# Scores of the first two tiles in free PSUM banks, tile 0 loaded in halves, and a new order of the first tiles

## The chip, the cores and the metric

The kernel runs on one core of one Trainium2 chip. The metric is the device time of one execution in microseconds. Engines are named as in the profile: PE (TensorE), DVE (VectorE), ACT (ScalarE), POOL (GpSimd), SP (the queue that issues most loads).

## The reference

Attention over 12 tiles of 128 queries (2 batches, 8 heads of 64, 6 tiles of a sequence of 768), where each query sees 8 global keys and the 96 positions up to its own, with a bias by distance; then a block with a softmax-like gate and a norm; then a block with SiLU:

```python
scores = scale * q @ k.T + bias            # masked by global and local windows
a = exp(scores - max); a = a / (sum(a) + 1e-9)
x = a @ v                                  # 1536 tokens x 512
h = x @ w_in                               # 512 -> 1024
e = exp(h - max(h)); solu = h * e / (sum(e) + 1e-9)
x = ((solu - mean) / sqrt(var + 1e-6) * g_ln) @ w_out     # 1024 -> 512
h = x @ w2_in                              # 512 -> 2048
out = (h * sigmoid(h)) @ w2_out            # 2048 -> 512
```

## The kernel before

Each engine has its own program, written out by hand, and the engines are tied by semaphores. A tile of 128 queries sees 232 keys (8 global, 96 before, its own 128). The eight heads form four pairs, so each step of attention exists four times per tile: `step(t, p)` for tile t and pair p. Where fp32 operands go through fast matmuls, they are split into a high and a low part (`_hi`, `_lo`), and three matmuls make one product.

For a tile of the attention the chain is: loads of keys and queries; on PE `early_scores(t, half)`, which makes two of the four pairs, four matmuls into the banks `score_ps[0]` and `score_ps[1]`; on DVE `mask(t, p)`, which adds the bias tables and finds the maximum; on ACT `exps(t, p)`; on DVE the reciprocals of the sums; on ACT or POOL `normalise`; on PE `turn_probs(t, p)` (four transposes); on ACT or DVE `copy_probs_t(t, p)`, out of the single bank `probs_t_ps`; on PE `values(t, p)` into `x_t_ps`. Then ACT's `x_high` and DVE's `x_low` split the result, and PE makes the hidden product: `hidden_by_rows(t, k)` for the first two tiles (six matmuls of 512 columns for each of four k, so that each needs one piece of `w_in` only), `hidden(t, n)` afterwards. On that follow `hidden_max` (DVE), `hidden_exp` (ACT), `hidden_solu` (DVE), `square` (ACT), `rstd` (POOL), `norm_u` (POOL or DVE), then on PE `turn_u(t, r)`, `project(t, r)`, and `turn_x1(t)`; `copy_x1` and `x1_high` are ACT's copies around it.

The bias tables of batch tile 0 come from ACT (`first_table(p)`), those of the other tiles from POOL (`late_table(p)`, four bias operations for two calls). Weights `w_in` and `w_out` are split in eight pieces: `split_w(n)` on ACT and DVE, `split_in_high(n)` and `low_w(n)` on POOL.

Before the regular loop `step(i)`, i from 4 on, each engine runs `first_steps()`, a list of such calls for tiles 0 to 3 and parts of tile 4 in a fixed order. An engine takes its list strictly in order, so a call that waits holds everything behind it. Each engine also has one branch, on a flag that is read from memory (`wide_flag`): a general path for other window sizes, not taken here. PE starts with `keep_warm`, matmuls on zeros whose result nobody reads.

SP issues the loads in order: tile 0's, tile 1's, values, `w_in` pieces, then, behind the branch, tile 2 (waits for the scores of tile 0), two pieces of `w_out`, tile 3 (waits for the scores of tile 1), two more, tile 4, values of tile 2, and the first loads of tile 5. ACT's queue issues half of tile 0's.

## Time and profile before

| | us |
|---|---|
| median of three runs | 494.79 (494.17 to 496.78) |
| the profiled execution | 493.58 |
| its span, first to last instruction | 491.5 |
| PE busy | 483.5 (98%) |
| DVE, ACT, POOL busy | 302.4, 269.7, 224.4 |

The timed runs and the profiled one are different executions of the same program. The span leaves out what lies before the first and after the last instruction of the program, 2.1 us here. Busy time of PE includes matmuls that overlap with the next one, so that the time from one start to the next tells more than the duration of one.

### The profile page before, as it was taken

The numbers are of one execution on the slowest core, as the hardware profiler recorded it, in microseconds if no ns is written. First come the engines' busy times: TensorE is split into PE (matmuls) and PEld (weight loads), VectorE is DVE, ScalarE is ACT, GpSimd is POOL, SyncE is SP. The second block draws the span as 40 slices with busy tenths as digits, with TensorE's granted clock in tenths as the row PEclk, the third lists the DMA queues.
The fourth block names the chain that finished last, engine by engine and source line by source line (L and its number), as shares of the span: only waits on it lengthen the run. The fifth ranks groups of instructions, "written<-read, shape, count | busy, mean of one in ns | idle before, by whom it ended". The sixth has DMA issues, their size and how long they took to land.

```text
span 491.5 us, 8017 instructions
## 1 busy us (share of the span) xinstructions
PE 483.5 (98%) x2761; PEld 414.2 (84%) x2761; DVE 302.4 (62%) x731; ACT 269.7 (55%) x598; POOL 224.4 (46%) x293
## 2 busy tenths in 40 slices
PE   8999999999999999999999999999999999999997
PEld 5667888888888878888898999988899998988995
DVE  5788665575675786666565667564565546545542
ACT  4988656576476465645845444455454454344422
POOL 6624207788778788530624422444135431444100
PEclk9999999999999999999999999999999999999999
DMA  8991021633532532302222202220116202220003
GB/s 239 299 260 49 18 66 37 159 82 79 159 101 61 159 105 57 125 0 87 86 87 87 82 6 85 85 87 31 55 65 237 86 4 83 87 85 1 1 1 128
DMA packets 20202, 44.38 MB, mean 90 GB/s; under 512 B 2560, under 2 KB 8128, under 8 KB 20160
## 3 DMA queue, kind: packets, MB, share of 16 engines
q1 hardware_dynamic: 20000, 43.47, 29.4%
q8 instruction: 23, 0.38, 0.3%
q10 hardware_dynamic: 160, 0.37, 0.3%
q14 instruction: 19, 0.16, 0.1%
HBM read 40.69 MB, written 3.15 MB: 89 GB/s over the span
## 4 chain that ended last, share of the span: by engine, by line
PE 68%; POOL 18%; issue 4%; DVE 4%; DMA 3%; ACT 1%; SPq 1%; POOLq 0%; DVEq 0%; ACTq 0%
PE hidden_ps L1162 24%; PE score_ps L1185 9%; POOL k_split L687 6%; PE x_ps L995 6%; POOL probs L714 5%; PE x_t_ps L1185 5%; PE x_ps L1185 5%; PE probs_t_ps L1185 5%; PE turn_ps L1185 4%; PE hidden_ps L950 3%; POOL k_split L685 3%; DVE solu L1738 2%; POOL q_lo L701 2%; DMA w_out_raw<-w_out 2%; PE score_ps L892 2%
## 5 line engine op out<-in xcount | busy, mean ns | idle before, releaser
L853 POOL TENSOR_TENSOR wo_lo<-w_raw,wo_hi 128x512 fp32r<-128x512 f32 x32 | 41.4, 1313 | 145.6 <-ACT wo_hi L1434 145.6
L1446 ACT ACTIVATE act_hi<-mix_c 128x384 fp32r<-128x384 f32 x64 | 33.7, 526 | 96.5 <-DVE mix_c L1827 96.2
L714 POOL TENSOR_SCALAR probs<-probs,exp_inv 128x232 f32<-128x232 f32 x80 | 35.4, 460 | 51.7 <-DVE exp_inv L1597 48.6
L1265 ACT ACTIVATE probs<-logits,low_logit 128x232 f32<-128x232 f32 x96 | 45.5, 478 | 3.4 <-DVE low_logit L1584 2.7
L1827 DVE TENSOR_TENSOR mix_u<-hidden_ps,mix_p 128x384 f32<-128x384 f32 x16 | 8.9, 558 | 57.0 <-PE hidden_ps L1162 57.0
L995 PE MATMUL x_ps<-w_out_hi,u_hi 128*128 128x512 f32 x96 | 40.6, 423 | 0.0
L1832 DVE TENSOR_TENSOR act_lo<-mix_c,act_hi 128x384 fp32r<-128x384 f32 x64 | 36.1, 566 | 6.3 <-ACT mix_c L1447 5.5
L995 PE MATMUL x_ps<-w_out_hi,u_lo 128*128 128x512 f32 x96 | 38.0, 395 | 0.0
L995 PE MATMUL x_ps<-w_out_lo,u_hi 128*128 128x512 f32 x96 | 37.5, 390 | 0.0
L1584 DVE CUSTOM_DVE_ANT_0 logits<-score_ps,bias 128x232 f32<-128x232 f32 x96 | 33.5, 395 | 2.3 <-issue 2.3
L950 PE MATMUL hidden_ps<-w_in_hi,x_hi 128*128 128x512 f32 x80 | 33.1, 414 | 0.0
L1447 ACT ACTIVATE mix_c<-mix_c 128x384 f32<-128x384 f32 x64 | 32.6, 509 | 0.0
L950 PE MATMUL hidden_ps<-w_in_hi,x_lo 128*128 128x512 f32 x80 | 31.5, 394 | 0.0
L950 PE MATMUL hidden_ps<-w_in_lo,x_hi 128*128 128x512 f32 x80 | 31.2, 390 | 0.0
L903 PE MATMUL probs_t_ps<-identity,probs 128*116 128x128 f32 x192 | 29.2, 274 | 0.2 <-ACT probs_t L1272 0.2
L1798 DVE TENSOR_TENSOR wa_lo<-w_sums,wa_hi 128x1024 fp32r<-128x1024 f32 x16 | 19.6, 1224 | 13.7 <-ACT wa_hi L1426 13.7
L903 PEld LDWEIGHTS probs_t_ps<-identity,probs 128*116 128x116 f32 x192 | 22.1, 134 | 6.6 <-issue 2.3
L1613 DVE TENSOR_TENSOR u_lo<-turn_ps,u_hi 128x512 fp32r<-128x512 f32 x24 | 16.5, 688 | 18.1 <-ACT u_hi L1279 18.1
L1162 PE MATMUL hidden_ps<-late_x_hi,wa_lo 128*128 128x384 f32 x80 | 27.1, 339 | 0.0
L1162 PE MATMUL hidden_ps<-late_x_hi,wa_hi 128*128 128x384 f32 x80 | 27.0, 337 | 0.0
L1162 PE MATMUL hidden_ps<-late_x_lo,wa_hi 128*128 128x384 f32 x80 | 27.0, 337 | 0.0
L1311 ACT ACTIVATE expd<-hidden_ps,stat 128x1024 f32<-128x1024 f32 x12 | 13.4, 1115 | 24.5 <-DVE stat L1651 24.5
(205 smaller groups left out, 1456.4 us busy)
## 6 DMA issues: line engine op xcount, KB each, us to landing
w_raw<-w SPq DMA_DIRECT2D x16, 1024.0 KB, 4.9
v_sb<-v_win SPq DMA_DIRECT2D x22, 224.0 KB
late_k_raw<-k_t SPq DMA_DIRECT2D x16, 232.0 KB, 4.0
k_raw<-k_t SPq DMA_DIRECT2D x14, 232.0 KB, 3.6
out<-out_sb SPq DMA_DIRECT2D x12, 256.0 KB, 2.1
w_in_raw<-w_in SPq DMA_DIRECT2D x4, 512.0 KB, 6.8
w_out_raw<-w_out SPq DMA_DIRECT2D x4, 512.0 KB, 10.5
late_q_raw<-q_t SPq DMA_DIRECT2D x16, 128.0 KB, 3.9
```

What stands on the lines that cost most here:

```text
L714: last = nc.gpsimd.tensor_scalar(probs[p][:, e, :], probs[p][:, e, :], exp_inv[:, p, e:e + 1], 0.0, ALU.mult, ALU.add)
L853: nc.gpsimd.tensor_tensor(wo_lo[j % 2][:, c, :], w2_raw[j % 2][:, c, BANK:2 * BANK], wo_hi[j % 2][:, c, :].bitcast(F32), ALU.subtract).the ...
L903: last = nc.tensor.transpose(probs_t_ps[0:HALF_KEYS, n * P:(n + 1) * P], probs[p][:, e, c * HALF_KEYS:(c + 1) * HALF_KEYS], identity[:, :])
L950: last = nc.tensor.matmul(hidden_ps[:, n * BANK:(n + 1) * BANK], x[:, k * P:(k + 1) * P], w[:, k, n * BANK:(n + 1) * BANK], start=(k == 0 ...
L995: last = nc.tensor.matmul(x1_ps[:, :], u[:, c * P:(c + 1) * P], w[:, c, :], start=(c == 0 and m == 0), stop=(c == KF - 1 and m == 2))
L1162: last = nc.tensor.matmul(dst, w[b][:, w_slot, cols], x[:, k, :], start=(k == 0 and m == 0), stop=(k == 1 and m == 2))
L1185: last = nc.tensor.matmul(out_ps[n][:, :], a[c][:, i * P:(i + 1) * P], w[b][:, chunk, :], start=(opens and m == 0), stop=(closes and m == 2))
L1265: last = nc.scalar.activation(probs[p][:, e, :], logits[b][:, e, :], ACT.Exp, scale=-1.0, bias=low_logit[:, b, e:e + 1], accum_out=exp_sum ...
L1446: nc.scalar.activation(act_hi[c][:, :], mix_c[c][:, :], ACT.Silu)
L1447: nc.scalar.activation(mix_c[c][:, :], mix_c[c][:, :], ACT.Silu).then_inc(act_hi_done, 1)
L1584: last = nc.vector.tensor_tensor_reduce(logits[b][:, e, :], score_ps[b][:, e * KEYS:(e + 1) * KEYS], bias[0 if t % TILES_PER_BATCH == 0 el ...
L1832: nc.vector.tensor_tensor(act_lo[c][:, :], mix_c[c][:, :], act_hi[c][:, :].bitcast(F32), ALU.subtract).then_inc(act_lo_done, 1)
```

## The change

1. `early_scores` writes to `score_bank(t, p)`. For tiles 0 and 1 the eight pairs go to eight places: the two score banks, `x_t_ps`, `x1_ps`, the two halves of `hidden_ps`, and the score banks again. The scores of tile 1, half 0, wait for no mask; those of half 1 wait for the first two masks. Waits for masks now stand before the first real use of the borrowed banks (`values(0, 0)`, `hidden_by_rows(0, 0)`, `project(0, 0)`). The warm-ups write to `turn_ps`.
2. `load_first` loads tile 0 in two halves of columns, from SP and from ACT, eight transfers in place of four, with a semaphore for each half.
3. `mask(0, 1)` stands in front of DVE's branch, `early_scores(0, 1)` in front of PE's. POOL's fill of the far part of the bias is divided: two heads early, six behind the flag.
4. The warm-ups start on a quarter of the zeros, made by POOL: five matmuls of 128 columns, then seven of 512 instead of nine; later 8 in place of 14, two of which had been full fp32.
5. All engines get a new order for the first tiles. Some steps change their engine: `norm_u(2)` goes from DVE to POOL; high parts of `w_in` 0 and 2 go from ACT to POOL; low parts of 0 and 1 from POOL to DVE, of 3 from DVE to POOL; copies and normalisations of some pairs swap.

Of DVE's new list the diff below shows only the ends.

```diff
+    early_score_ps = [*score_ps, x_t_ps, x1_ps, hidden_ps[:, 0:BANK], hidden_ps[:, BANK:2 * BANK], *score_ps]
...
+    def score_bank(t, p):
+
+        return early_score_ps[PAIRS * t + p] if t < 2 else score_ps[p % 2]
...
-    ACT_NORMALISES = ((0, 0), (0, 1), (1, 2), (1, 3), (2, 3), (3, 0), (3, 2), (3, 3))
-    POOL_NORMALISES = ((0, 2), (0, 3), (1, 1), (1, 0), (2, 0), (2, 1), (2, 2), (3, 1))
-    ACT_WEIGHTS = (2, 0, 3, 4, 5, 6, 7)
-    POOL_WEIGHTS = (1,)
-    POOL_LOWS = (0, 1)
+    ACT_NORMALISES = ((0, 0), (1, 1), (1, 2), (2, 2), (3, 1), (3, 3))
+    POOL_NORMALISES = ((0, 1), (0, 2), (0, 3), (1, 0), (1, 3), (2, 0), (2, 1), (2, 3), (3, 0), (3, 2))
+    ACT_WEIGHTS = (3, 4, 5, 6, 7)
+    POOL_WEIGHTS = (0, 2, 1)
+    POOL_LOWS = (3,)
...
+    def load_first(eng, unit):
+
+
+        rows = slice(unit * DH, unit * DH + DH)
+        for half, loaded in enumerate((first_half_loaded, early_loaded[0])):
+            keys = slice(half * 2 * KEYS, (half + 1) * 2 * KEYS)
+            queries = slice(half * 2 * P, (half + 1) * 2 * P)
+            eng.dma_start(staged_k_raw[rows, keys], k_v[0, unit][:, keys]).then_inc(loaded, 16)
+            eng.dma_start(staged_q_raw[rows, queries], q_v[0, unit][:, queries]).then_inc(loaded, 16)
...
-            load_early(0)
+            load_first(sp, 1)
             load_early(1)
...
+            nc.gpsimd.memset(x_hi[:, 0:P].bitcast(F32), 0.0).then_inc(first_zeros_made, 1)
...
-            nc.gpsimd.memset(bias[0][:, :, 0:BEFORE], -BIG / SCALE).then_inc(far_made, 1)
+            nc.gpsimd.memset(bias[0][:, 0:2, 0:BEFORE], -BIG / SCALE).then_inc(far_made, 1)
...
             flag()
+            nc.gpsimd.memset(bias[0][:, 2:HEADS, 0:BEFORE], -BIG / SCALE).then_inc(far_made, 1)
             with pool.If(wide_flag(pool) > 0):
...
             late_distances()
+            normalise(0, 1)
             late_table(0)
             late_table(1)
+            normalise(0, 2)
+            split_in_high(0)
+            normalise(0, 3)
             late_table(2)
             late_table(3)
-            normalise(0, 2)
+            normalise(1, 0)
+            split_in_high(2)
             split_in_high(1)
-            normalise(0, 3)
-            normalise(1, 1)
-            normalise(1, 0)
-            low_w(0)
-            low_w(1)
+            low_w(3)
+            normalise(1, 3)
             normalise(2, 0)
             normalise(2, 1)
-            normalise(2, 2)
+            normalise(2, 3)
+            normalise(3, 0)
             rstd(0)
             norm_u(0)
-            normalise(3, 1)
+            normalise(3, 2)
+            rstd(1)
+            normalise(4, 0)
             normalise(4, 1)
-            normalise(4, 0)
-            rstd(1)
             rstd(2)
+            norm_u(2)
...
-                if half == 0:
+                if t == 0 and half == 0:
+                    pe.wait_ge(first_half_loaded, 64)
+                elif t == 0 or half == 0:
                     pe.wait_ge(early_loaded[t], 64)
-                after(pe, masked_done, PAIRS * t + 2 * half)
+                if t > 1:
+                    pe.wait_ge(masked_done, PAIRS * t + 2 * half)
+                elif (t, half) == (1, 1):
+                    pe.wait_ge(masked_done, 2)
...
-                        last = nc.tensor.matmul(score_ps[unit][:, e * KEYS:(e + 1) * KEYS], queries[rows, h * P:(h + 1) * P],
+                        dst = score_bank(t, 2 * half + unit)[:, e * KEYS:(e + 1) * KEYS]
+                        last = nc.tensor.matmul(dst, queries[rows, h * P:(h + 1) * P],
...
+                if (t, p) == (0, 0):
+                    pe.wait_ge(masked_done, 3)
...
+                if t == 0 and k == 0:
+                    pe.wait_ge(masked_done, PAIRS + 2)
...
+                    if t == 0 and r == 0:
+                        pe.wait_ge(masked_done, PAIRS)
...
+                    nc.tensor.matmul(turn_ps[:, :], x_hi[:, 0:P], x_hi[:, :], start=True, stop=True)
...
-                keep_warm(2)
-                keep_warm_whole(2)
-                early_scores(0, 1)
-                keep_warm(8)
+                keep_warm(4)
+                early_scores(1, 0)
+                early_scores(1, 1)
                 turn_probs(0, 0)
-                keep_warm(2)
-                early_scores(1, 0)
+                keep_warm(4)
                 turn_probs(0, 1)
                 values(0, 0)
                 turn_probs(0, 2)
-                early_scores(1, 1)
                 values(0, 1)
                 turn_probs(0, 3)
                 values(0, 2)
                 values(0, 3)
                 turn_probs(1, 0)
+                turn_probs(1, 1)
+                hidden_by_rows(0, 0)
                 early_scores(2, 0)
-                turn_probs(1, 1)
                 values(1, 0)
-                hidden_by_rows(0, 0)
+                values(1, 1)
                 hidden_by_rows(0, 1)
+                early_scores(2, 1)
+                turn_probs(1, 2)
                 hidden_by_rows(0, 2)
                 hidden_by_rows(0, 3)
-                turn_probs(1, 2)
-                early_scores(2, 1)
-                values(1, 1)
                 turn_probs(1, 3)
+                early_scores(3, 0)
+                turn_probs(2, 0)
                 values(1, 2)
                 values(1, 3)
-                turn_probs(2, 0)
-                early_scores(3, 0)
+                early_scores(3, 1)
                 turn_probs(2, 1)
+                values(2, 0)
+                turn_probs(2, 2)
+                values(2, 1)
                 hidden_by_rows(1, 0)
-                values(2, 0)
-                early_scores(3, 1)
+                values(2, 2)
+                turn_probs(2, 3)
                 hidden_by_rows(1, 1)
-                values(2, 1)
-                turn_probs(2, 2)
+                turn_probs(3, 0)
+                values(2, 3)
+                turn_u(0, 0)
+                turn_probs(3, 1)
                 hidden_by_rows(1, 2)
-                turn_probs(2, 3)
-                values(2, 2)
                 hidden_by_rows(1, 3)
-                turn_u(0, 0)
-                values(2, 3)
-                turn_probs(3, 0)
+                turn_u(0, 1)
+                turn_probs(3, 2)
                 early_scores(4, 0)
-                turn_u(0, 1)
+                turn_probs(3, 3)
                 project(0, 0)
-                turn_probs(3, 1)
+                all_values(3)
                 project(0, 1)
-                turn_probs(3, 2)
                 hidden(2, 0)
-                turn_probs(3, 3)
+                turn_u(1, 0)
                 hidden(2, 1)
-                turn_u(1, 0)
-                all_values(3)
                 turn_u(1, 1)
                 project(1, 0)
-                early_scores(4, 1)
                 turn_x1(0)
                 project(1, 1)
+                early_scores(4, 1)
...
+            pe.wait_ge(first_zeros_made, 1)
+            for _ in range(5):
+                nc.tensor.matmul(turn_ps[:, 0:P], x_hi[:, 0:P], x_hi[:, 0:P], start=True, stop=True)
             pe.wait_ge(zeros_made, 1)
-            keep_warm(9)
+            keep_warm(7)
             early_scores(0, 0)
+            early_scores(0, 1)
...
 
                 first_table(2)
+                first_table(3)
                 exps(0, 1)
-                first_table(3)
                 early_normalise(0, 0)
                 exps(0, 2)
-                early_normalise(0, 1)
                 exps(0, 3)
                 copy_probs_t(0, 1)
                 exps(1, 0)
+                copy_probs_t(0, 2)
                 exps(1, 1)
-                split_w(2)
-                split_w(0)
-                split_w(3)
+                copy_probs_t(0, 3)
+                early_normalise(1, 1)
                 exps(1, 2)
                 x_high(0)
+                split_w(3)
+                copy_probs_t(1, 1)
                 exps(1, 3)
                 split_w(4)
                 exps(2, 0)
+                early_normalise(1, 2)
                 exps(2, 1)
                 split_w(5)
-                early_normalise(1, 2)
-                early_normalise(1, 3)
+                exps(2, 2)
+                copy_probs_t(1, 2)
+                copy_probs_t(1, 3)
+                exps(2, 3)
+                hidden_exp(0)
+                x_high(1)
+                early_normalise(2, 2)
+                copy_probs_t(2, 1)
+                exps(3, 0)
+                exps(3, 1)
+                square(0)
+                early_normalise(3, 1)
+                exps(3, 2)
+                exps(3, 3)
+                copy_probs_t(3, 0)
+                early_normalise(3, 3)
+                u_high(0, 0)
                 split_w(6)
-                hidden_exp(0)
-                copy_probs_t(1, 3)
-                exps(2, 2)
-                x_high(1)
-                copy_probs_t(2, 0)
-                exps(2, 3)
-                exps(3, 0)
-                early_normalise(2, 3)
-                copy_probs_t(2, 1)
                 split_w(7)
-                square(0)
-                copy_probs_t(2, 2)
-                exps(3, 1)
-                exps(3, 2)
-                early_normalise(3, 0)
-                u_high(0, 0)
                 x_high(2)
+                copy_probs_t(3, 2)
+                u_high(0, 1)
                 hidden_exp(1)
-                u_high(0, 1)
-                exps(3, 3)
+                copy_probs_t(3, 3)
                 exps(4, 0)
+                square(1)
                 exps(4, 1)
-                early_normalise(3, 2)
-                early_normalise(3, 3)
-                square(1)
                 copy_x1(0)
-                copy_probs_t(3, 2)
                 u_high(1, 0)
-                hidden_exp(2)
                 x_high(3)
                 u_high(1, 1)
+                hidden_exp(2)
+                x1_high(0)
                 square(2)
-                x1_high(0)
                 copy_x1(1)
...
-            act.dma_start(staged_k_raw[0:DH, :], k_v[0, 0]).then_inc(early_loaded[0], 16)
-            act.dma_start(staged_q_raw[0:DH, :], q_v[0, 0]).then_inc(early_loaded[0], 16)
+            load_first(act, 0)
...
-            nc.vector.memset(x_hi[:, :].bitcast(F32), 0.0).then_inc(zeros_made, 1)
+            nc.vector.memset(x_hi[:, P:BANK].bitcast(F32), 0.0).then_inc(zeros_made, 1)
...
-                norm_u(2)
                 x1_low(0)
...
             mask(0, 0)
+            mask(0, 1)
             with dve.If(wide_flag(dve) > 0):
```

PE behind its branch, up to the first product with values. The banks and `probs_63` to `probs_66` (pairs 0 to 3) are named with their buffer numbers. Before:

```order
L1034 MATMUL x_ps<-x_hi 128x512 x2
L1039 MATMUL x_ps<-x_hi 128x512 x2
L892 MATMUL score_ps<-staged_k_raw,staged_q_raw 128x232 x4
L1034 MATMUL x_ps<-x_hi 128x512 x8
L903 MATMUL probs_t_ps<-identity,probs_63 116x128 x4
L1034 MATMUL x_ps<-x_hi 128x512 x2
L892 MATMUL score_ps<-next_k_raw,next_q_raw 128x232 x4
L903 MATMUL probs_t_ps<-identity,probs_64 116x128 x4
L937 MATMUL x_t_ps<-probs_t_67,v_sb_59 64x128 x4
```

and now:

```order
L1067 MATMUL turn_ps<-x_hi 128x512 x4
L919 MATMUL hidden_ps<-next_k_raw,next_q_raw 128x232 x4
L919 MATMUL score_ps<-next_k_raw,next_q_raw 128x232 x4
L930 MATMUL probs_t_ps<-identity,probs_63 116x128 x4
L1067 MATMUL turn_ps<-x_hi 128x512 x4
L930 MATMUL probs_t_ps<-identity,probs_64 116x128 x4
L966 MATMUL x_t_ps<-probs_t_67,v_sb_59 64x128 x4
L930 MATMUL probs_t_ps<-identity,probs_65 116x128 x4
L966 MATMUL x_t_ps<-probs_t_68,v_sb_60 64x128 x4
```

The scores of tile 0's second half are gone from here (they stand ahead of the branch), all scores of tile 1 stand ahead of the first turn, and eight warm-ups are left of fourteen.

ACT at the end of its list, from the exponential of tile 2's hidden row (`expd,stat<-hidden_ps`) on; `expd,stat<-solu` is `square(2)`, `x_f` and `own_x_hi` are the two operations of `x1_high(0)`, `x_sb` is `copy_x1`. Before:

```order
L1311 ACTIVATE expd,stat<-hidden_ps,stat 128x1024
L1307 ACTIVATE x_hi<-x_t_ps 128x512
L1279 ACTIVATE u_hi<-turn_ps 128x512
L1316 ACTIVATE expd,stat<-solu,stat 128x1024
L1391 ACTIVATE x_f_118<-turn_ps 128x4x128
L1393 ACTIVATE own_x_hi<-turn_ps 128x4x128
L1382 ACTIVATE x_sb<-x_ps 128x512
```

and now (the list shown begins with `u_high(1, 0)`):

```order
L1308 ACTIVATE u_hi<-turn_ps 128x512
L1336 ACTIVATE x_hi<-x_t_ps 128x512
L1308 ACTIVATE u_hi<-turn_ps 128x512
L1340 ACTIVATE expd,stat<-hidden_ps,stat 128x1024
L1420 ACTIVATE x_f_118<-turn_ps 128x4x128
L1422 ACTIVATE own_x_hi<-turn_ps 128x4x128
L1345 ACTIVATE expd,stat<-solu,stat 128x1024
L1411 ACTIVATE x_sb<-x_ps 128x512
```

`square(2)` stood ahead of `x1_high(0)` and now stands behind it; both `u_high` of tile 1 now stand ahead of the exponential.

POOL at the same place, around the entry of the regular loop; `stat<-stat` pairs are `rstd`, the rows into `solu` are `norm_u`. Before:

```order
L714 TENSOR_SCALAR probs_64<-probs_64,exp_inv 128x232 x4
L714 TENSOR_SCALAR probs_63<-probs_63,exp_inv 128x232 x2
L722 TENSOR_SCALAR stat<-stat 128x1
L724 TENSOR_TENSOR stat<-stat 128x1
L722 TENSOR_SCALAR stat<-stat 128x1
L724 TENSOR_TENSOR stat<-stat 128x1
L714 TENSOR_SCALAR probs_65<-probs_65,exp_inv 128x232 x2
L714 TENSOR_SCALAR probs_66<-probs_66,exp_inv 128x232 x2
```

and now:

```order
L730 TENSOR_SCALAR probs_63<-probs_63,exp_inv 128x232 x2
L730 TENSOR_SCALAR probs_64<-probs_64,exp_inv 128x232 x2
L738 TENSOR_SCALAR stat<-stat 128x1
L740 TENSOR_TENSOR stat<-stat 128x1
L804 TENSOR_TENSOR stat<-stat 128x1
L805 TENSOR_TENSOR stat<-stat 128x1
L807 TENSOR_SCALAR solu<-solu,stat 128x1024
L730 TENSOR_SCALAR probs_65<-probs_65,exp_inv 128x232 x2
L730 TENSOR_SCALAR probs_66<-probs_66,exp_inv 128x232 x2
```

`norm_u(2)`, with its two small operations, has come in front of tile 4's pairs 2 and 3.

## Rows read from the trace of the kernel before

**Rows 1.** The page: PE's share, then two groups (count, busy us, mean ns).

```profile
PE 483.5 (98%) x2761; PEld 414.2 (84%) x2761; DVE 302.4 (62%) x731; ACT 269.7 (55%) x598; POOL 224.4 (46%) x293
...
L1265 ACT ACTIVATE probs<-logits,low_logit 128x232 f32<-128x232 f32 x96 | 45.5, 478 | 3.4 <-DVE low_logit L1584 2.7
...
L1584 DVE CUSTOM_DVE_ANT_0 logits<-score_ps,bias 128x232 f32<-128x232 f32 x96 | 33.5, 395 | 2.3 <-issue 2.3
```

**Rows 2.** Busy us of each engine by stretch, then clock, DMA share and GB/s.

```profile
0.00:24.44 24.44, 21.32 (x130) 14.15 (x130) 15.93 (x76) 16.72 (x52) 16.72 (x42) 1.00 0.97 269
24.44:72.44 48.00, 46.98 (x310) 36.53 (x309) 36.08 (x112) 34.21 (x87) 11.17 (x22) 1.00 0.38 94
72.44:200.00 127.56, 126.89 (x863) 106.67 (x862) 84.14 (x259) 76.64 (x202) 100.77 (x122) 1.00 0.38 102
```

**Rows 3.** Waits of PE: who waited for whom, us in total, times, longest.

```profile
PE x_t_ps L937 <- ACT probs_t L1272: 1.0, 1, 1.0
...
PE score_ps L877 <- POOL q_lo L701: 0.4, 2, 0.2
```

**Rows 4.** Timeline to 24.5 us: start, us, engine, line, operation, count, idle before it.

```profile
1.46 4.21 PE L1034 MATMUL x_ps<-x_hi 128*128 128x512 f32 x9 [1.46 <-DVE x_hi L1526]
...
5.96 1.78 PE L892 MATMUL score_ps<-staged_k_raw,staged_q_raw 64*128 64x232 f32 x8 [0.30 <-DMA staged_q_raw<-q_t]
...
7.91 0.06 DVE L1582 MEMSET wait_mark<- 128x1 f32 x1 [2.00 <-PE score_ps L892]
...
9.79 0.06 DVE L1582 MEMSET wait_mark<- 128x1 f32 x1 [1.11 <-issue]
...
11.60 2.12 PE L1034 MATMUL x_ps<-x_hi 128*128 128x512 f32 x8
...
20.80 0.66 PE L937 MATMUL x_t_ps<-probs_t,v_sb 116*64 116x128 f32 x8 [0.45 <-DVE probs_t L1609]
...
24.44 0.50 PE L965 MATMUL hidden_ps<-w_in_hi,x_hi 128*128 128x512 f32 x1
```

**Rows 5.** DMA view of the first 50 us: issues, KB, us from issue to landing.

```profile
staged_q_raw<-q_t ACTq DMA_DIRECT2D x1, 128.0 KB, 4.1
...
spans_i<-spans SPq DMA_DIRECT2D x1, 2.0 KB, 1.6
```

**Rows 6.** DMA view of issues at 24.4 and 26.9 us; busy by stretch, 2 to 36.

```profile
late_q_raw<-q_t SPq DMA_DIRECT2D x1, 128.0 KB, 12.0
...
k_raw<-k_t SPq DMA_DIRECT2D x1, 232.0 KB, 10.6
...
2.00:36.00 34.00, 31.31 (x201) 21.71 (x201) 25.20 (x104) 26.71 (x77) 18.51 (x38) 1.00 1.05 282
```

**Rows 7.** Timeline of `norm_u(0)` on POOL, then of 62.4 to 72.5 us.

```profile
44.74 1.19 POOL L790 TENSOR_SCALAR solu<-solu,stat 128x1024 f32<-128x1024 f32 x1
...
62.37 0.60 PE L978 MATMUL turn_ps<-identity,solu 128*128 128x128 f32 x4
...
62.57 1.22 DVE L1651 TENSOR_REDUCE stat<-hidden_ps 128x1 f32<-128x1024 f32 x1 [2.04 <-PE hidden_ps L950]
...
63.83 1.11 ACT L1311 ACTIVATE expd<-hidden_ps,stat 128x1024 f32<-128x1024 f32 x1 [0.22 <-DVE stat L1651]
...
65.65 1.22 DVE L1658 CUSTOM_DVE_ANT_0 solu<-hidden_ps,expd 128x1024 f32<-128x1024 f32 x1 [1.26 <-PE turn_ps L978]
...
67.44 1.24 ACT L1316 ACTIVATE expd<-solu,stat 128x1024 f32<-128x1024 f32 x1 [1.29 <-DVE stat L1665]
...
68.20 1.05 PE L892 MATMUL score_ps<-late_k_raw,late_q_raw 64*128 64x232 f32 x8
...
68.86 0.19 POOL L722 TENSOR_SCALAR stat<-stat 128x1 f32<-128x1 f32 x1 [10.04 <-ACT expd L1316]
...
69.88 0.60 ACT L1391 ACTIVATE x_f<-turn_ps 128x512 f32<-128x512 f32 x1 [1.11 <-PE turn_ps L1007]
...
69.98 0.81 DVE L1738 TENSOR_SCALAR solu<-solu,stat 128x1024 f32<-128x1024 f32 x1
...
72.44 0.60 PE L978 MATMUL turn_ps<-identity,solu 128*128 128x128 f32 x4
```

74 lines of the change are left out of this document (33 added, 41 removed).

## The prediction

> **What bounds the kernel now.** First the page: TensorE (PE) is busy for 98% of the span [rows 1]. A share over the whole span hides where it is not, so next the busy time by stretch [rows 2]. The cut at 24.44 us is the first matmul of the first block's hidden product, the cut at 72.44 us the first instruction of the regular loop `step(4)`, which the change leaves alone. From 24.44 to 72.44 us PE works 46.98 of 48.00 us, in the stretch behind it 126.89 of 127.56 us. Only before 24.44 us is there more room, and part of the 21.32 busy us there is warm-up matmuls on zeros that compute nothing. The view of waits then names what PE stood still for [rows 3]: 1.0 us once for a copy of turned probabilities, and in the loop 0.4 us for GpSimd's (POOL's) split of the queries. So the loop is paced by PE itself with POOL close behind: each iteration starts from PE's `turn_u`, ACT's and POOL's work hangs on it, and all moves with it. The change is worth exactly what it takes off the start of `step(4)`, now 72.44 us.
>
> The order before that start is read from the timeline [rows 4]: nine warm-ups from 1.46 us, scores of tile 0 at 5.96, their mask at 7.91, the second mask after a hole of 1.11 us (the branch), and the hidden product at 24.44.
>
> **Start of PE (gain).** The first half of the columns is half of tile 0's bytes, so it can land before the warm-ups are through. Then these set the start. The nine take 4.21 us, 0.43 us from one start to the next. The change begins them on a shorter memset at about 1.1 us, issues five short ones (0.1 to 0.2 us each, by a quarter of the columns) and seven long ones (7 x 0.43 = 3.0): 1.1 + 0.2 + 0.8 + 3.0 = 5.1 us for `early_scores(0, 0)`, 0.9 sooner. If the half came late (a transfer issued in that stretch took 4.1 us, the smallest 1.6 [rows 5]; the last first-half piece is issued at 1.8 us, so 3.4 to 5.9), it would be between 5.1 and 5.96. I take 5.1.
>
> **From there to the hidden product (gain).** A mask is two operations of 0.4 us, exponentials for a pair of heads two of 0.48 [rows 1]. Step by step: `mask(0, 0)` 7.05 to 7.75, `mask(0, 1)` to 8.45 without the branch between them; the branch's 1.1 us now stands behind both, so `mask(0, 2)` comes at 9.55 + 0.35 for reciprocals = 9.9. ACT does `exps(0, 0)` to 8.75, two tables to 9.7, `exps(0, 1)` to 10.7, `early_normalise(0, 0)` to 11.5, `exps(0, 2)` to 12.4, `exps(0, 3)` to 13.35. DVE's reciprocals of pair 2 wait for 12.4, and the copy of pair 0 stands behind them: it is done at 13.5. PE's `turn_probs(0, 1)` thus starts at 13.55, pair 2 at 14.85, pair 3 at 16.4 (ACT does three of the four copies now, one behind the other with exponentials between), and `values(0, 3)` ends at 18.55 (21.4 before: it starts at 20.80 [rows 4]). The scores of tile 1 wait for no mask of tile 0 any more and lie in holes of PE; they cost it nothing here, since PE then waits for ACT. POOL has pushed the tables of tile 1 and two weight pieces between normalisations and delivers pair 0 of tile 1 at 19.0, then come a turn, a copy on DVE and `x_low(0)`: **the hidden product starts at about 21.15 us**. Before, PE had by 24.44 also done `early_scores(2, 0)` and `values(1, 0)` (1.0 + 0.6), which now come later: like for like 22.85 against 21.15, a gain of 1.7 us. The new waits for `masked_done` in front of `values(0, 0)`, `project(0, 0)` and `hidden_by_rows(0, 0)` guard banks whose masks are done 3 us or more before; I cost them at nothing. What pays for the gain is slack on PE, so it costs nothing if the walk is 0.5 us off either way.
>
> **The floor.** With no wait behind it: 21.15 + 1.6 + 46.98 = 69.75 us for `step(4)`, against 72.44: 2.7 us, and no order of the same work gives more.
>
> **The values of tile 2 (loss).** From 2 to 36 us the DMA queues are full (share 1.05, 282 GB/s), so what lands late is set by the bytes ahead of it and not by its issue, and the change keeps the order of all loads behind tile 0. `v_sb` for tile 2 lies between the last `late_q_raw` piece, issued at 24.4 and landed 12.0 us later at 36.4, and the first `k_raw` piece, issued at 26.8 and landed 10.6 later at 37.4 [rows 6]. Before, `values(2, 0)` came at 38.6, behind both. Now PE's work from 21.15 to it is 24 hidden matmuls (24 x 0.231 = 5.55), four halves of scores (3.9), four turns (2.3) and four `values` (2.4): 14.15, so PE asks at 35.3 and waits until 36.4 to 37.4. I take 1.2 us, bounds 0.3 (if the landings came 0.8 sooner) and 2.1. Note that this wall also swallows any error in the start: PE arriving later waits less.
>
> **The norm in front of `step(4)` (loss).** `turn_u(2, 0)` needs `norm_u(2)`, and that the end H of `hidden(2, 1)`. Now it is 62.37, and the chain runs [rows 7]: maximum at +0.2 for 1.22, exponential at +1.46 for 1.2, `hidden_solu` 1.22 and three small ones 0.57, square 1.33, POOL's two 0.82, DVE's norm 1.1: ended at 70.8, 1.65 us before PE asks at 72.44. In the change PE has less left after H: turn 0.44, two projections of 2.77, a turn 0.45, and scores 1.0, together 7.45 us where it was 10.07. The chain gets longer: mean ready at H + 4.5; `square(2)` now stands behind `x1_high(0)` on ACT, which starts when `turn_x1(0)` is through (H + 3.9) and takes 1.1 us (the first of its two operations is in [rows 7]), so square starts at H + 5.05 and ends at 6.4; POOL's two end at 7.3; `norm_u(2)`, now on POOL, takes 1.19 and two small ones (0.38 with their waits 0.45) and ends at H + 9.0. PE arrives at H + 7.45 and waits 1.55 us (bounds 1.0 and 2.2). H is the floor less 7.45 plus the values' wait: 69.75 - 7.45 + 1.2 = 63.5. So **`step(4)` starts at 63.5 + 9.0 = 72.5 us, where it starts now**, with `exps(4, 2)` and POOL's work following `turn_u(2, 0)` as before.
>
> **Sum.** -1.7 (early stages) - 1.0 (the copy wait that goes, [rows 3]) + 1.2 + 1.55 = +0.05 us. The profiled execution took 493.58 us, 2.1 more than its span of 491.5; the three timed ones 494.17, 494.79 and 496.78. The middle of the four is 494.5, and I forecast **494.5 us**. What a measurement of this kernel can tell from no change is about 0.5%, 2.5 us.
>
> **Rivals.** (a) *One of the two late waits isn't there.* If `v_sb` landed before PE asks, `step(4)` would start 1.2 us sooner; if the norm kept ahead of PE, 1.55 sooner: 493.3 or 492.95. For it: bytes can be served in another order by queues filled earlier. Against: the queue's share shows no hole to use, and the order on ACT and POOL is fixed. (b) *Both are gone:* the floor, 2.7 us less, 491.8. (c) *One more wait* between 10 and 60 us of about 1 us, where I found an answer ready within 0.3 us of its use (`turn_probs(1, 3)` behind two copies and a weight split on ACT): 495.5. (d) *The clock falls back, slower.* The nine first warm-ups run at 0.43 us each, the lower of TensorE's two levels (1.2 GHz), though the granted clock reads 1.00; the eight at 11.60 us run at 0.23, the upper one (2.4 GHz) [rows 4]. The change issues 15 long warm-ups instead of 23 and leaves PE six holes of 0.1 to 0.6 us between 11 and 21 us, in place of the warm-ups at 11.60. Scores of half a tile took 1.78 us at the lower level and 1.05 at the upper [rows 4, 7], 1.7 times as long. If the clock fell in those holes, six turns and four products (0.6 us each) would take 0.7 x 6.0 = 4.2 us more, less 1.8 us of holes that they fill, and the first eight hidden matmuls 0.2 us more each: 2.4 + 1.6 = 4.0 us, 498.5. [...] The trace of before has one wait of PE of 1.0 us [rows 3] with matmuls at full rate behind it. The Trainium skill, "TensorE: Matmul & The Clock Gate", section "The HAM clock gate", has the array throttled by default and released by activity; by that rule the thinner start is a risk, and the trace agrees that the first matmuls run at half speed.
>
> **How the numbers follow.** Forecast 0.58; (a) 0.20; (b) 0.06; (c) 0.10; (d) 0.06. Faster by over 0.5%: (b) and a tail of the spread, 0.07. Slower by over 0.5%: (d) and a little, 0.07. Within 0.5%: 0.86. The range holds forecast, (a) and (c) with a spread of some 0.8 us: 492.1 to 496.5; it leaves out (b) and (d) and little more.
>
> **What the profile will show.** Right: first scores at about 5.1 us, hidden product near 21.1, a wait of about 1 us of the tile-2 `values` for a DMA, a wait of about 1.5 us of `turn_u` for POOL's `solu`, `step(4)` at 72.5. Wrong in the early stages: a hidden product after 22. Wrong in the late ones: no wait for `solu`, `step(4)` before 71.5. Wrong as a whole: matmuls of 512 columns at 0.43 us after 12 us, or new waits in the loop behind `step(4)`.

## The result and the profile after

The changed kernel is slower. Median 500.39 us (498.8 to 502.67, 7 runs) against 494.79 us (494.06 to 496.78, 7 runs); the ratio is 1.0106, 95% interval [1.0077, 1.0136]. Timed a second time beside others it was 1.0130 [1.0088, 1.0172]. The forecast was 494.5 us, in a range up to 496.5.

The busy time by stretch of the changed kernel, cut at the first hidden matmul (23.31 us), at the first instruction of `step(4)` (81.89 us), and 127.56 us behind it, as long as the third stretch of [rows 2] (start:end, length, then busy us of PE, PE's weight loads, DVE, ACT, POOL with counts, granted clock, DMA share, GB/s):

```profile
0.00:23.31 23.31, 17.58 (x108) 12.64 (x109) 14.57 (x69) 13.37 (x45) 16.60 (x44) 0.90 0.91 232
23.31:81.89 58.58, 52.26 (x326) 39.96 (x325) 37.00 (x114) 36.81 (x91) 17.08 (x30) 0.92 0.39 90
81.89:209.45 127.56, 126.85 (x863) 106.75 (x864) 83.98 (x257) 76.18 (x201) 100.80 (x122) 1.00 0.39 106
```

The loop behaves as before: in 127.56 us PE works 126.85 us on 863 matmuls, 126.89 on 863 in [rows 2]. All the loss lies before it. `step(4)` starts at 81.89 us in place of 72.44, 9.45 us later, and the span is 500.9 in place of 491.5, 9.4 us longer. In the second stretch the clock reads 0.92 where it was 1.00. What PE stood still for (who waited for whom, us in total, times, longest; `next_q_raw` are the queries of tile 1, `staged_q_raw` here those of tile 2):

```profile
PE x_t_ps L966 <- DMA v_sb<-v_win: 3.1, 1, 3.1
PE probs_t_ps L930 <- POOL probs L730: 2.2, 1, 2.2
PE turn_ps L1009 <- POOL solu L807: 1.3, 1, 1.3
PE hidden_ps L919 <- DMA next_q_raw<-q_t: 1.2, 1, 1.2
...
PE score_ps L919 <- DMA staged_q_raw<-q_t: 1.0, 1, 1.0
```

And the places in the timeline of PE (start, us, operation, count, idle before it and its releaser):

```profile
5.38 1.05 PE L919 MATMUL score_ps<-staged_k_raw,staged_q_raw 64*128 64x232 f32 x8
...
11.57 0.65 PE L930 MATMUL probs_t_ps<-identity,probs 128*116 128x128 f32 x4
...
17.94 0.65 PE L930 MATMUL probs_t_ps<-identity,probs 128*116 128x128 f32 x4 [2.19 <-POOL probs L730]
...
23.31 0.78 PE L996 MATMUL hidden_ps<-w_in_hi,x_hi 128*128 128x512 f32 x1
23.88 0.63 PE L996 MATMUL hidden_ps<-w_in_lo,x_hi 128*128 128x512 f32 x1
...
43.97 1.13 PE L966 MATMUL x_t_ps<-probs_t,v_sb 116*64 116x128 f32 x8 [3.15 <-DMA v_sb<-v_win]
```

The start is as forecast to 0.3 us (scores at 5.38, forecast 5.1; first turn at 11.57, forecast 11.5). `turn_probs(0, 3)` comes at 17.94 and not at 16.4, the hidden product at 23.31 and not at 21.15. The values of tile 2 come at 43.97, where the forecast had their load at 36.4 to 37.4. The granted clock falls twice: the first time 0.8 us behind the wait that ends at 17.94, the second time within the wait that ends at 43.97 (same columns as the stretches above):

```profile
16.00:18.80 2.80, 0.86 (x8) 0.69 (x10) 1.82 (x5) 0.92 (x5) 2.72 (x5) 0.99 1.01 326
18.80:25.50 6.70, 5.79 (x29) 4.29 (x26) 4.66 (x13) 4.60 (x13) 4.46 (x7) 0.50 1.06 210
25.50:42.80 17.30, 13.41 (x100) 9.39 (x98) 14.16 (x49) 13.03 (x40) 6.88 (x9) 0.99 1.04 236
42.80:49.60 6.80, 5.63 (x26) 3.98 (x26) 2.29 (x13) 3.57 (x11) 2.00 (x7) 0.51 0.06 21
```

0.50 is the lower level, 1.2 GHz. A matmul of 512 columns starts 0.43 us after the one ahead there (23.88, then 24.31), 0.23 us at the upper level. The first fall is rival (d), to which the forecast gave 6%.

The other new thing is the transfers. From 2 to 36 us the kernel before moved 282 GB/s at a share of 1.05 [rows 6]. In the same stretch the changed one moves 248 GB/s, with the engines hardly less busy:

```profile
2.00:36.00 34.00, 27.34 (x166) 19.38 (x165) 24.29 (x97) 22.49 (x70) 21.30 (x41) 0.90 1.02 248
```

Of `w_in_raw` the first piece, issued at 6.81 us before and at 8.09 now, and the last `late_q_raw` piece (issued at 25.03 us; [rows 6] has 12.0), from issue to landing:

```profile
w_in_raw<-w_in SPq DMA_DIRECT2D x1, 512.0 KB, 6.7
```

```profile
late_q_raw<-q_t SPq DMA_DIRECT2D x1, 128.0 KB, 18.1
```

The first took 5.0 us before. So an issue 1.28 us later lands 3.0 us later at 14.8 us, and one 0.7 us later lands 6.8 us later at 43.1 us.

### The profile page after: what moved, and what is told of

Its sections match the earlier page's. It is cut to its first block, busy times and chain, and to the rows that moved or that the text cites. A ratio compares the mean times of both kernels' runs of the same rounds, so it can differ in the third digit from the quotient of the medians.

```text
span 500.9 us, 8013 instructions
## 1 busy us (share of the span) xinstructions
PE 484.9 (97%) x2756; PEld 416.0 (83%) x2756; DVE 301.7 (60%) x725; ACT 268.4 (54%) x596; POOL 230.3 (46%) x303
## 3 DMA queue, kind: packets, MB, share of 16 engines
HBM read 40.69 MB, written 3.15 MB: 88 GB/s over the span
## 4 chain that ended last, share of the span: by engine, by line
PE 64%; POOL 18%; SPq 5%; issue 4%; DVE 3%; DMA 3%; ACT 1%; POOLq 0%; ACTq 0%
PE hidden_ps L1191 24%; PE score_ps L1214 9%; POOL k_split L703 6%; PE x_ps L1028 5%; POOL probs L730 5%; PE x_t_ps L1214 4%; PE x_ps L1214 4%; PE probs_t_ps L1214 4%; PE turn_ps L1214 4%; DMA v_sb<-v_win 3%; PE hidden_ps L979 3%; POOL k_split L701 3%; DVE solu L1761 2%; POOL q_lo L717 2%; PE x_t_ps L966 1%
## 5 line engine op out<-in xcount | busy, mean ns | idle before, releaser
L874 POOL TENSOR_TENSOR wo_lo<-w_raw,wo_hi 128x512 fp32r<-128x512 f32 x32 | 41.4, 1312 | 145.9 <-ACT wo_hi L1463 145.9
L730 POOL TENSOR_SCALAR probs<-probs,exp_inv 128x232 f32<-128x232 f32 x84 | 39.5, 488 | 44.3 <-DVE exp_inv L1625 42.4
L1028 PE MATMUL x_ps<-w_out_hi,u_hi 128*128 128x512 f32 x96 | 40.6, 422 | 0.0
L1028 PE MATMUL x_ps<-w_out_hi,u_lo 128*128 128x512 f32 x96 | 37.8, 394 | 0.0
L930 PE MATMUL probs_t_ps<-identity,probs 128*116 128x128 f32 x192 | 30.7, 284 | 4.2 <-POOL probs L730 2.2
L1612 DVE CUSTOM_DVE_ANT_0 logits<-score_ps,bias 128x232 f32<-128x232 f32 x88 | 30.5, 395 | 4.0 <-issue 4.0
L930 PEld LDWEIGHTS probs_t_ps<-identity,probs 128*116 128x116 f32 x192 | 22.7, 139 | 11.8 <-POOL probs L730 3.8
L966 PE MATMUL x_t_ps<-probs_t,v_sb 116*64 116x128 f32 x352 | 25.2, 291 | 3.2 <-DMA v_sb<-v_win 3.1
L966 PEld LDWEIGHTS x_t_ps<-probs_t,v_sb 116*64 116x64 f32 x352 | 20.4, 143 | 8.5 <-issue 5.1
```

Source lines behind the costliest of these rows:

```text
L730: last = nc.gpsimd.tensor_scalar(probs[p][:, e, :], probs[p][:, e, :], exp_inv[:, p, e:e + 1], 0.0, ALU.mult, ALU.add)
L874: nc.gpsimd.tensor_tensor(wo_lo[j % 2][:, c, :], w2_raw[j % 2][:, c, BANK:2 * BANK], wo_hi[j % 2][:, c, :].bitcast(F32), ALU.subtract).the ...
L930: last = nc.tensor.transpose(probs_t_ps[0:HALF_KEYS, n * P:(n + 1) * P], probs[p][:, e, c * HALF_KEYS:(c + 1) * HALF_KEYS], identity[:, :])
L966: last = nc.tensor.matmul(x_t_ps[e * DH:(e + 1) * DH, at:at + P], values_of(t, s)[:, c, h * DH:(h + 1) * DH], probs_t_of(t, p)[:, (2 * e + ...
L1028: last = nc.tensor.matmul(x1_ps[:, :], u[:, c * P:(c + 1) * P], w[:, c, :], start=(c == 0 and m == 0), stop=(c == KF - 1 and m == 2))
```

## Experiments

Each kernel was timed against the kernel before on the same chip (the chips differ from one group of kernels to another). In the table "step(4)" is the start of its first turn on PE in the profiled execution, "q lands" the landing of the last `late_q_raw` piece (what stands next ahead of `v_sb` of tile 2), "low" whether the clock reads 0.50 anywhere after 10 us.

| kernel | ratio [95%] | step(4), us | q lands, us | low |
|---|---|---|---|---|
| before; again | 1; 1.0002 [0.9975, 1.0029] | 72.44; 74.26 | 36.4; 38.3 | no |
| after; again | 1.0106; 1.0130 | 81.89; 81.87 | 43.1; 43.0 | twice |
| a_whole | 1.0018 [1.0003, 1.0033] | 75.93 | 37.6 | 18 to 28 |
| b_start | 1.0061 [1.0041, 1.0082] | 76.22 | 39.4 | 19 to 29 |
| a_warm | 1.0067 [1.0040, 1.0095] | 79.23 | 42.5 | 22 to 26 |
| a_rows | 1.0056 [1.0028, 1.0083] | 80.29 | 42.6 | twice |
| w_pool | 1.0012 [0.9995, 1.0029] | 75.64 | 38.3 | 24 to 27 |
| w_best | 1.0012 [0.9991, 1.0032] | 75.40 | 39.0 | 23 to 27 |
| a_delay | 1.0075 [1.0043, 1.0107] | 78.52 | 42.4 | 21 to 28 |
| a_actq | 1.0043 [1.0021, 1.0065] | 77.10 | 39.7 | 8 to 15, 25 to 28 |
| b_whole | 1.0017 [0.9993, 1.0040] | 74.99 | 38.8 | 24 to 28 |
| b_delay | 1.0057 [1.0035, 1.0080] | 77.47 | 40.6 | 24 to 32 |
| w_warm | 1.0007 [0.9984, 1.0030] | 75.06 | 37.9 | no |
| b_warm | 1.0000 [0.9981, 1.0019] | 73.65 | 38.4 | no |
| a_w0 | 1.0106 [1.0066, 1.0145] | 77.33 | 41.0 | 14 to 17 |
| b_early | 1.0046 [1.0024, 1.0068] | 75.54 | 39.8 | 10 to 14 |

In every row the span less the start of `step(4)` is 419.0 to 419.2 us (before 491.5 - 72.44 = 419.1; after 500.9 - 81.89 = 419.0; b_warm 492.7 - 73.65 = 419.1). So one number of the trace stands for the whole time of that execution, as the forecast had it. It is one execution, and not always a typical one: the profiled run of a_rows took 501.2 us and its median is 498.3, of a_w0 498.3 and 499.9, of b_start 497.2 and 498.8.

The rate of the loads from 8 to 38 us divides the kernels, with the share at 1.04 to 1.06 in all of them. The kernel before moves 284 and 279 GB/s in its two traces. The six with whole loads of tile 0 and SP's loads of tile 1 issued from 2.4 us on (a_whole, w_pool, w_best, b_whole, w_warm, b_warm) move 271 to 277. The change moves 249 and 244, and the other eight, with halves, rows or shifted issues, 242 to 268.

**Both kernels again.** Do the slow transfers belong to the change?

> The changed kernel a second time, with a second trace. Its first trace moved 10 MB of loads at about 240 GB/s from 8 to 42 us where the kernel before moved them at about 290, and v_sb of tile 2 landed at 43.9 us. Theory L (the slow transfers belong to the change): the second trace shows the same rate within 3%, the same wait for v_sb of 3 us and the same two stretches at clock 0.50; ratio 1.010 to 1.013. Theory V (the rate varies from one execution to the next): another rate, v_sb landing 2 us or more earlier or later, and a span that moves with it.

> The kernel before a second time. Theory L: 290 GB/s from 8 to 38 us as in the first trace, k_raw landing at 37 us, span 491 to 492. Theory V: a rate that differs by more than 5% from the first trace's, but hardly a longer span, since in this order nothing stands close to its transfer.

They do. The stretches from 8 to 14 us of the kernel before (again), and of the changed kernel in its first trace:

```profile
8.00:14.00 6.00, 5.82 (x28) 3.48 (x26) 3.35 (x22) 5.35 (x21) 4.03 (x11) 1.00 1.07 320
```

```profile
8.00:14.00 6.00, 4.82 (x37) 3.43 (x37) 4.24 (x28) 5.08 (x21) 3.85 (x10) 1.00 1.03 271
```

The second trace of the change has 274, the same two falls of the clock and `step(4)` at 81.87. The kernel before varies more than I had thought: its second trace starts `step(4)` at 74.26, after a wait of 2.0 us for tile 2's queries. It stands closer to its transfers than its first trace showed.

**Whole loads, and the old order with halves.**

```diff
-        for half, loaded in enumerate((first_half_loaded, early_loaded[0])):
...
+        eng.dma_start(staged_k_raw[unit * DH:unit * DH + DH, :], k_v[0, unit]).then_inc(early_loaded[0], 16)
+        eng.dma_start(staged_q_raw[unit * DH:unit * DH + DH, :], q_v[0, unit]).then_inc(early_loaded[0], 16)
```

> The changed kernel with tile 0's keys and queries loaded whole again (four transfers, not eight); everything else as changed. Theory L with the halves as cause (64 more packets of half the size on each of two queues, and four more issues that push every later one back by 1.28 us): the rate goes back to about 290 GB/s, v_sb of tile 2 lands at 37 us, ratio below 1.003. If the halves only start PE sooner: the first scores 0.5 us later and all else the same, ratio 1.010 to 1.013.

> The changed kernel with the order of the first tiles, and the division of normalisations and weight splits between the engines, as before: only the banks, the halves, the first masks ahead of the branch and the shorter warm-ups are left of the change. Theory O (the new order costs: PE stands behind v_sb, behind POOL's split of a weight piece that waits for its transfer, and behind POOL's norm, and twice falls to the lower clock): ratio 0.995 to 1.000, no stretch at clock 0.50 after 12 us. Theory W (the thinner start loses the clock whatever the order): clock 0.50 somewhere between 12 and 25 us, ratio above 1.004.

Whole loads alone take the ratio from 1.0106 and 1.0130 to 1.0018: the halves make most of the loss. The rate from 8 to 14 us is back at 322 GB/s, the wait for `v_sb` is gone, `step(4)` starts at 75.93, 6 us sooner. But `v_sb` did not land at 37 us. In a_whole PE, late by its lower clock, asks for it at 40.21. Three later kernels with whole loads ask sooner and all wait until 40.2 (w_pool, w_best, w_warm; here w_best):

```profile
40.15 0.67 PE L957 MATMUL x_t_ps<-probs_t,v_sb 116*64 116x128 f32 x8 [0.77 <-DMA v_sb<-v_win]
```

Why that is still 3 us behind the forecast is taken up in the next section. In the old order the halves cost 1.0061 against 1.0017 (b_whole, below), with `step(4)` at 76.22 against 74.99. Of my two theories for b_start the second is nearer: its clock did fall.

**More warm-ups; and the same bytes cut another way.** a_warm puts ten warm-ups ahead of `turn_probs(0, 3)` and fourteen matmuls on a finished piece of `w_in_hi` ahead of `values(2, 0)`:

```diff
+                keep_warm(10)
                 turn_probs(0, 3)
...
+                keep_warm_late(14)
                 values(2, 0)
```

> The changed kernel with more matmuls that compute nothing, in the two places where PE stood still for 2 us and more ahead of a fall of the clock: ten of 512 columns (0.23 us each) ahead of turn_probs(0, 3), fourteen ahead of the first values of tile 2; halves and order as changed. Theory K (the clock falls because PE stands still, and costs about 2.5 us in each of the two stretches): no stretch at clock 0.50 after 12 us, the same transfers (v_sb of tile 2 near 43 us), the step(4) turn 3 to 5 us sooner than 81.9, ratio about 1.003. Theory N (the waits alone set the time, since what PE does at the lower clock would wait anyway): clock back, and less than 1 us gained, ratio 1.010 or more.

The wait for `v_sb` is covered by the fourteen, the second fall of the clock is gone, a fall of 3.4 us is left (22.5 to 25.9 us), and `step(4)` comes 2.65 us sooner. The values of tile 2 start at nearly the same time:

```profile
43.74 0.67 PE L966 MATMUL x_t_ps<-probs_t,v_sb 116*64 116x128 f32 x8
```

From there to `step(4)` are 35.5 us (35.5 in a_delay too, which has no fall there either) and 37.9 in the change. So the second fall cost 2.4 us. That is theory K, though less than the 3 to 5 us and the ratio of 1.003 that it expected.

a_rows loads tile 0 in eight transfers of 32 whole rows each, so that the number of transfers is as in the change, but not the size of a packet. An issue of 32 rows takes SP 0.42 us in place of 0.60, so its later loads come 0.6 us later than with whole loads, not 1.28:

```diff
+            rows = slice(unit * DH + half * DH // 2, unit * DH + (half + 1) * DH // 2)
+            part = slice(half * DH // 2, (half + 1) * DH // 2)
+            eng.dma_start(staged_k_raw[rows, :], k_v[0, unit][part, :]).then_inc(early_loaded[0], 16)
```

> The changed kernel with tile 0 loaded in eight transfers as in the change, but cut by rows (32 rows of full length each) and not by columns, so that each packet has its full size; PE waits for all. Theory S (the smaller packets put the engines out of step): rates and landings as with whole loads, ratio 1.002. Theory Q (four transfers more in the queues and every later issue 1.28 us later): about 270 GB/s from 8 to 14 us, v_sb of tile 2 at 43 us, ratio about 1.011.

q lands at 42.6 us and PE waits 2.0 us for `v_sb`. So the slow transfers need no small packets, and no delay of 1.28 us either. The ratio, 1.0056, lies between the two theories; its ten runs go from 496.2 to 501.4 us.

**Later issues alone.** Of the four transfers more, two are SP's, and they push its later issues back by 1.28 us. a_delay keeps whole loads and lets SP wait in that place for a step of DVE's table; b_delay puts the same line into the kernel before (its edit is shown). The first weight piece is issued 1.1 us later by it in a_delay and 1.5 us later in b_delay:

```diff
             load_early(0)
+            sp.wait_ge(table_step, 5)
             load_early(1)
```

> The changed kernel with whole loads of tile 0 (four transfers; ratio 1.0018), and SP waits for the fifth step of DVE's table (about 3.65 us) ahead of the loads of tile 1: every later issue comes about 1.3 us later, as in the change, with no transfer and no packet more. Theory I (the queues run short between 2 and 8 us because the issues come too late, and the engines stay out of step after it): a DMA share below 0.95 from 2 to 8 us, 270 to 290 GB/s from 8 to 14 us where whole loads had 322, v_sb of tile 2 near 43 us, ratio 1.006 to 1.011. Theory M (more transfers, not later ones, cost it): rate 320 GB/s from 8 to 14 us, every landing at most 1.3 us later, ratio 1.002 to 1.004.

> The kernel before with one wait added: SP waits for the fifth step of DVE's table (3.65 us) behind the loads of tile 0, so every later issue comes 1.3 us later. Theory I (late issues slow all transfers that follow): last landings of the weight pieces and of tile 4's loads 3 to 5 us later than before, not 1.3; ratio 1.003 or more, since this order has its values of tile 2 at 38.6 us and would now wait for them. Rival: the slow transfers need the change's order; every landing 1.3 us later, ratio 0.999 to 1.003.

The wait alone is enough, in both orders: 1.0018 becomes 1.0075, and 1 becomes 1.0057. The ten runs of a_delay lie far apart (496.5 to 503.9 us), so what the delay sets off is not the same in each. In its trace q lands at 42.4, and PE waits:

```profile
PE x_t_ps L959 <- DMA v_sb<-v_win: 2.2, 1, 2.2
```

In b_delay the rate is that of the change, and the scores of tile 2 wait 2.7 us for their load, then the clock falls for most of 24 to 32 us:

```profile
8.00:14.00 6.00, 5.50 (x27) 3.42 (x26) 3.77 (x24) 4.77 (x19) 4.04 (x11) 1.00 0.96 275
```

```profile
PE score_ps L893 <- DMA staged_q_raw<-q_t: 2.9, 2, 2.7
```

How the delay does it is less clear. My theory I, that the queues run short between 2 and 8 us, had a_delay at 270 to 290 GB/s from 8 to 14 us. It had 317:

```profile
8.00:14.00 6.00, 6.00 (x36) 4.39 (x33) 3.96 (x27) 4.94 (x21) 2.17 (x6) 1.00 1.04 317
...
32.00:38.00 6.00, 5.74 (x36) 4.07 (x32) 4.82 (x19) 5.20 (x18) 2.75 (x4) 1.00 1.08 208
```

and fell behind only later, to 208 GB/s. In a_delay a transfer's last part comes far behind. The last two `late_q_raw` pieces are issued 0.64 us apart and land 5.2 us apart, in a_whole 2.7 (from issue to landing, first and second piece; a_whole, then a_delay):

```profile
late_q_raw<-q_t SPq DMA_DIRECT2D x1, 128.0 KB, 13.2
...
late_q_raw<-q_t SPq DMA_DIRECT2D x1, 128.0 KB, 15.3
```

```profile
late_q_raw<-q_t SPq DMA_DIRECT2D x1, 128.0 KB, 13.3
...
late_q_raw<-q_t SPq DMA_DIRECT2D x1, 128.0 KB, 17.9
```

The same within one transfer: the 16 signals by which the last piece of `w_out` tells of its landing come over 8.0 us in a_delay, over 3.4 in a_whole. The Trainium skill, "DMA: Bandwidth & Descriptors", section "Two DMAs through the same engine are not ordered", says that nothing orders the transfers across the 16 engines. That they get out of step is what the landings of a_delay look like. It is not the mark of every slow kernel: those 16 signals come over 6.2 and 4.9 us in the change's two traces, 5.5 in b_delay and 3.3 in b_start, against 3.2 and 4.5 in the kernel before and 5.0 in w_best, which is not slow. So it is not shown to be the cause. Why a delay of 1.1 us sets off the loss of rate, and why it lasts for 30 us, no run here shows.

**Keep the halves, mend the issues?** a_actq lets ACT issue both second halves, so that SP's later loads start at 2.4 us again; a_w0 loads weight piece 0 ahead of tile 1, to fill the queue sooner.

> The changed kernel with the halves kept, but ACT issues both second halves: SP issues two transfers of tile 0 as before, and its later loads start at 2.4 us, not 3.7. Theory I: DMA share near 1.00 from 2 to 8 us, 310 GB/s or more from 8 to 14 us, v_sb of tile 2 at 38 to 39 us, ratio 1.001 to 1.004. Theory M: 270 GB/s, v_sb at 42 us or later, ratio about 1.010.

> The changed kernel, halves and order as changed, with weight piece 0 (512 KB with one issue of 0.35 us) loaded ahead of tile 1's keys and queries and not behind tile 0's values. If the queue running short is the cause: DMA share near 1.00 from 2 to 8 us, over 300 GB/s from 8 to 14 us, v_sb of tile 2 near 39 us in place of 43, ratio 1.001 to 1.004 against 1.011 to 1.013 (tile 1's loads land 1.5 us later, which PE's warm-ups cover in part). Rival (any issue behind 3 us is too late, however full the queue): 270 GB/s and v_sb at 43 us, ratio 1.010 or more.

a_actq: q lands at 39.7, there is no wait for `v_sb`, but tile 0's second half lands late and PE stands still ahead of it:

```profile
PE x_t_ps L918 <- DMA staged_q_raw<-q_t: 3.6, 1, 3.6
```

The ratio 1.0043 is 0.006 to 0.009 below the change's. Its `v_sb` was there at 41.4 us, later than the 40.1 of whole loads, with SP's issues on time. So a_delay shows that the delay is enough, and a_rows and a_actq leave open what the four transfers more add to it. a_w0 did not test what it was made for: its share from 2 to 8 us stayed at 0.86, since the large transfer still came behind all halves. PE waits 3.0 us for tile 1's queries, q lands at 41.0, and the ratio did not move. Whether a full queue would make the halves free stays open.

**What the new order costs by itself.** With whole loads, w_pool puts `normalise(0, 3)` ahead of `split_in_high(0)` on POOL. w_best besides puts `square(2)` back ahead of `x1_high(0)`, `norm_u(2)` back on DVE, and adds three warm-ups.

```diff
-            split_in_high(0)
             normalise(0, 3)
+            split_in_high(0)
```

> The changed kernel with whole loads of tile 0 (ratio 1.0018 before), and on POOL normalise(0, 3) ahead of the split of weight piece 0, not behind it. Theory K (PE's 1.7 us hole at 17 us is what lets the clock fall): pair 3 ready 2 us sooner, the hole is gone, no or a shorter stretch at 0.50, step(4) 3 us sooner than 75.9, ratio about 0.996. Theory T (the whole thin stretch from 10 to 18 us does it, not this one hole): the fall stays, 1 to 2 us gained at most, ratio 0.998 to 1.000.

> As the run with whole loads and normalise(0, 3) ahead of the weight split, and besides square(2) back ahead of x1_high(0), norm_u(2) back on DVE, and ten warm-ups ahead of the first scores in place of seven. The norm chain then ends within 0.3 us of PE's turn: the wait of 1.27 us for POOL's solu goes; ratio 0.0025 below that run's. Rival: the norm on DVE keeps u_low or a mask of tile 4 waiting, and the 1.27 us come back as a wait in step(4): no difference.

The hole moves and stays as large. In a_whole PE waited 1.7 us for POOL's `probs` ahead of `turn_probs(0, 3)`; in w_pool it waits for POOL one pair later:

```profile
21.80 0.65 PE L922 MATMUL probs_t_ps<-identity,probs 128*116 128x128 f32 x4 [2.02 <-POOL probs L724]
```

POOL has two normalisations, four bias operations and a split to do either way. In w_best the wait of 1.27 us for the norm becomes one of 1.03 us, put down to DVE (`own_x_lo`). The norm's last operation and `x1_low(0)` on DVE, and the turn on PE behind them:

```profile
73.84 0.81 DVE L1753 TENSOR_SCALAR solu<-solu,stat 128x1024 f32<-128x1024 f32 x1
74.57 0.68 DVE L1767 TENSOR_TENSOR own_x_lo<-turn_ps,own_x_hi 128x512 fp32r<-128x512 f32 x1
...
75.40 0.63 PE L1000 MATMUL turn_ps<-identity,solu 128*128 128x128 f32 x4 [1.03 <-DVE own_x_lo L1767]
```

The norm now ends at 74.65, 0.75 us ahead of the turn, but `turn_u` writes the bank that `x1_low` reads, and `x1_low` now stands behind the norm. This is the rival in another place: a new wait in front of `step(4)` takes back most of the old one, and the ratio is 1.0012 for both kernels. The three warm-ups had no chance to show in it: both kernels start the values of tile 2 as soon as `v_sb` lands, at 40.16 and 40.15 us.

**Without any fall of the clock.** b_whole is the old order with the banks, the early masks and the new start of the warm-ups. b_warm adds to it three warm-ups ahead of the first scores, six ahead of the first turn and six small ones ahead of the scores of tile 2. w_warm adds small ones to w_best in the two holes ahead of tile 1's turns, and puts `norm_u(2)` behind `x1_low(0)`.

> Whole loads of tile 0, the order and the division of work as before; of the change only the banks, the first two masks ahead of the branch and the start of the warm-ups are left. If the halves were what cost this order its 3 us (ratio 1.0061): ratio 0.996 to 1.001. If the thinner warm-ups did (ten long ones fewer ahead of the second mask, clock 0.50 from 19 to 29 us in the run with halves): the fall stays and the ratio is 1.003 or more.

> The changed order with whole loads, normalise(0, 3) ahead of the weight split, norm_u(2) on DVE behind x1_low(0), and ten small matmuls that compute nothing in the two holes of PE ahead of the turns of tile 1. If the clock is what still costs this order (0.50 from 23 to 27 us in the run without them: eight hidden matmuls at 0.43 us in place of 0.23): the fall goes, 1.5 us less, and the wait of 1.03 us ahead of step(4) shrinks to 0.3: ratio 0.996 to 0.999. Rival: tile 2's loads and its v_sb, which land at 23 and 39 us whatever PE does, take all of it back: ratio 1.000 to 1.002.

> The order before with the change's banks and first masks ahead of the branch, whole loads, ten warm-ups ahead of the first scores, fourteen ahead of the first turn and six small ones ahead of the scores of tile 2, where PE waits 2.6 us for a load. If the clock (0.50 from 24 to 28 us) was what ate the earlier start: ratio 0.995 to 0.999. Rival: the scores of tile 2 wait for their load at 23.5 us in this order whatever comes ahead, so that an earlier start is worth nothing: ratio 0.999 to 1.002 with the clock at 1.00.

The clock stays up in both (w_warm, then b_warm):

```profile
10.00:30.00 20.00, 16.45 (x134) 12.14 (x132) 15.78 (x59) 14.55 (x48) 13.77 (x22) 1.00 1.05 278
```

```profile
10.00:30.00 20.00, 17.41 (x129) 12.84 (x128) 15.06 (x61) 17.27 (x52) 11.35 (x17) 1.00 1.05 288
```

and the ratios are 1.0007 [0.9984, 1.0030] and 1.0000 [0.9981, 1.0019]. Banks, early masks and new order are worth nothing that can be measured, with every fall of the clock taken out. This is w_warm's rival: PE waits for `v_sb` until 40.18 us, as in w_pool and w_best, so all that it gained ahead of that is lost. In all it still waits 5.6 us behind its start, never over 0.9 us at a time, for `v_sb` 0.8; in b_warm 1.4 us for tile 2's queries and 1.9 for ACT and DVE. b_whole kept its fall at 24 us, as its second case had it, but lost less by it than expected there (1.0017 for 1.003).

**Still earlier?** In b_early ACT issues all of tile 0, and SP begins with tile 1 at 1.2 us.

> The order before with banks, early masks and more warm-ups (ratio 1.000), and all four whole transfers of tile 0 issued by ACT, so that SP begins tile 1's loads at 1.2 us and not at 2.4. If earlier issues win in the same way as later ones lose: all landings 1 us sooner or more, ratio 0.996 to 0.999. Rival (the queues are full from 2.4 us on already): landings of tile 2 and later as they were, tile 0's 1 us later, since tile 1's share the rate, and ratio 1.000 to 1.003.

Worse, 1.0046: PE waits 2.6 us for tile 0, whose transfers now run beside tile 1's. Nothing later landed sooner (q at 39.8, in b_warm 38.4), and the rate from 8 to 38 us is 267 GB/s in place of 274, though SP issued its loads 1.2 us sooner. So a later issue is not the only thing that lowers the rate.

## Why the prediction was wrong

**Bound: right.** The change was worth what it did to the start of `step(4)`, in all 18 traces to 0.2 us. The floor of 69.75 us was never reached: with every fall of the clock taken out the start is 73.65 (b_warm) or 75.06 us (w_warm).

**Start of PE: right.** 5.38 us against 5.1, and the first turn at 11.57 against 11.5.

**The values of tile 2: the step that failed.** The prediction had `v_sb` land at 36.4 to 37.4 us and PE start on it at 36.5. It started at 43.97. That is 7.5 of the 9.45 us, and the landing was wrong by two things.

The first is the delay. The prediction said that "what lands late is set by the bytes ahead of it and not by its issue, and the change keeps the order of all loads behind tile 0". The 1.28 us by which SP's two new issues push the others back was not counted at all. With whole loads `v_sb` lands at 40.1 us (w_pool, w_best, w_warm), with the halves at 43.9 and, in the second trace, 43.7: 3.8 us. a_delay shows that a delay of 1.1 us by itself does most of this (42.9 us); whether the transfers more do the rest stays open.

The second is a reading. The view of [rows 6] gives no landing for `v_sb`, and the prediction put it between those of a load issued before it and one issued after it. The signals that `values(2, 0)` waits for, which the trace keeps, end at 37.8 us in that same trace, behind both, and at 39.3 us in the kernel before's second. With whole loads the new order has them at 40.1. So 3.7 us of the 7.5 are there without the halves too. They take back what the early stages win, and no run tried to get this load sooner.

PE itself was late too. It asked for `v_sb` at 40.82 and not at 35.3. So the wait, forecast at 1.2 us (bounds 0.3 and 2.1), was 3.15, and with `v_sb` on time PE would have started at 40.8 and no sooner. Of these 5.5 us 2.2 are the late hidden product (below), 1.9 are three waits behind it (0.95 for tile 2's queries, 0.67 for ACT's `probs` and 0.29 for a copy), and 1.2 are six matmuls at the lower clock. A late `v_sb` alone would have cost all 7.5 us, a late PE alone 4.3.

**The clock: right mechanism, wrong chance and size.** Rival (d) had one fall, in the holes of 11 to 21 us, at 4.0 us and 6%. There were two. The second, which came in the wait for `v_sb`, cost 2.4 us: from 43.97 to 81.89 are 37.9 us, against 35.5 in a_warm. By the trace the first fall cost nothing in the end, since PE waited 3.15 us for `v_sb` behind it; that was not tried apart.

**From the masks to the hidden product: 2.2 us too early.** POOL's `split_in_high(0)` waited 0.68 us for weight piece 0, which landed at 14.8 and not at 11.8, with `normalise(0, 3)` behind:

```profile
14.91 1.04 POOL L792 TENSOR_SCALAR w_in_hi<-w_in_raw 128x1024 fp32r<-128x1024 f32 x1 [0.68 <-DMA w_in_raw<-w_in]
15.93 1.96 POOL L730 TENSOR_SCALAR probs<-probs,exp_inv 128x232 f32<-128x232 f32 x2
```

The two operations of the normalisation took 1.96 us in place of 0.9. Over it lies DVE's low part of the same weight:

```profile
15.98 1.22 DVE L1587 TENSOR_TENSOR w_in_lo<-w_in_raw,w_in_hi 128x1024 fp32r<-128x1024 f32 x1 [1.42 <-POOL w_in_hi L792]
```

The last section comes back to it. The late weight is the smaller part: in a_whole the split waits for nothing, the normalisation still takes 1.79 us, PE waits 1.66 us for it, and the hidden product starts at 24.14 us. In w_warm, with whole loads, the other order on POOL and no fall of the clock, it starts at 23.42. So the walk was over 2 us too early for timely loads as well.

**The norm: right.** Forecast 1.55 us (bounds 1.0 and 2.2), measured 1.26.

**Sum.** +7.5 (start of the values of tile 2) + 2.4 (second fall of the clock) - 0.5 (the path behind, 35.5 us where the forecast had 36.0; 0.3 of it is the norm) + 0.05 (forecast) = 9.45 us in the profiled executions. The medians lie 5.6 us apart; the first trace of before was one of its faster ones (`step(4)` at 74.26 in the second, 1.8 us later), and the profiled run of the change, 502.67 us, was its slowest.

**The range** left out (d) and had no case for transfers that slow down together. It ended at 496.5, 3.9 us short.

## What to carry to other kernels

Where the queues are full, more issues ahead of a long row of loads aren't free: count each issue (1.28 us for two here), and test the delay alone, with one added wait, before the change is built. Where a view gives no landing for a load, don't take it from its neighbours; look for a wait on it, and at more than one trace. A wait of PE can cost twice, once as itself and once by the clock: falls came with waits of 1.66 (a_whole), 2.02 (w_pool), 2.19 and 3.15 us, and none with one of 2.0 us (before, again). Matmuls that compute nothing, put where PE stands still anyway, took the second fall away in a_warm and all of them in w_warm and b_warm; that is worth time only where no load sets the start of what follows. Moving one step past another on a loaded engine (w_pool, w_best) moved the wait to the next user and won nothing.

## What was not expected of the hardware

- A delay of 1.1 us in SP's issues from 2.4 us on made the last queries of tile 4, some 20 us further down SP's list, land 4.8 us later (a_delay: issued at 24.5 and landed at 42.4; in a_whole 22.4 and 37.6), with the same bytes and the same count of transfers. The share of the DMA engines was 1.06 and 1.08 while the rate fell from 267 to 252 GB/s (20 to 26 us) and from 238 to 208 (32 to 38 us).
- POOL and DVE hold each other up. In a_whole, one operation of POOL on 128x232 elements and DVE's subtraction of two inputs in SBUF:

```profile
16.30 1.21 DVE L1579 TENSOR_TENSOR w_in_lo<-w_in_raw,w_in_hi 128x1024 fp32r<-128x1024 f32 x1
```

```profile
16.48 1.36 POOL L724 TENSOR_SCALAR probs<-probs,exp_inv 128x232 f32<-128x232 f32 x1 [0.32 <-DVE exp_inv L1624]
```

  POOL's takes 0.46 us elsewhere (two in 0.90 us); here it ends 0.33 us behind DVE's. The Trainium skill, "SBUF — State Buffer", section "Who interferes with whom", says that a DVE instruction with two SBUF inputs contends with a POOL instruction that reads SBUF; the trace agrees. The other way round, a small DVE operation took 1.07 us beside POOL's split of a weight piece (15.11 to 16.16 us), where one of twice the elements takes 0.17 us behind it:

```profile
15.11 1.07 DVE L1622 TENSOR_SCALAR exp_den<-exp_sum 128x2 f32<-128x2 f32 x1
...
17.70 0.17 DVE L1615 TENSOR_SCALAR exp_den<-exp_sum 128x4 f32<-128x4 f32 x1 [0.19 <-ACT probs L1286]
```
